# Two pairs of casts on ScalarE and one normalisation on VectorE, moved to other places in a fused attention and expert kernel

## The reference

```
attn_out = softmax(mask(q k^T / 8)) v          # 4 x 8 heads, 576 positions, head size 64, mask by blocks of 64
x = attn_out as 2304 tokens x 512
p = domain_probs / (domain_probs.sum(-1) + 1e-9)     # 2304 x 4
for e in range(4):
    h = max(x @ w1[e], 0)                      # 2304 x 1024
    out += p[:, e:e+1] * (h @ w2[e])           # 2304 x 512
h = out @ w_in; solu = h * softmax(h); ln = layernorm(solu) * g_ln
return ln @ w_out                              # 2304 x 512
```

## Time and profile before

| what | value |
|---|---|
| median of 3 runs | 1162.6 us (1162.32 to 1163.42) |
| the profiled execution's own time | 1163.42 us |
| its span | 1161.6 us |
| PE busy | 1141.0 us (98%) |
| PEld busy | 1020.3 us (88%) |
| DVE busy | 643.9 us (55%) |
| ACT busy | 425.7 us (37%) |
| POOL busy | 415.1 us (36%) |
| longest wait of PE | 2.9 us, for the sum of line 1412 |

### The profile page before, as it was taken

One profiled execution on the slowest core, in us unless ns is written; L12 is line 12 of the kernel. 1 busy time (PEld: TensorE's weight loads), 2 busy tenths in 40 slices (PEclk: granted clock), 3 DMA queues, 4 the chain that ended last, 5 costly groups with the idle time before them and its releaser, 6 DMA issues.

```text
span 1161.6 us, 16745 instructions
## 1 busy us (share of the span) xinstructions
PE 1141.0 (98%) x6131; PEld 1020.3 (88%) x6131; DVE 643.9 (55%) x1155; ACT 425.7 (37%) x927; POOL 415.1 (36%) x403
## 2 busy tenths in 40 slices
PE   8999998989999999999999999999999999999998
PEld 7999898879999999999999999999999977888887
DVE  8999997544343534343433434352424468666765
ACT  7888785232213311113311112321112344434432
POOL 7998896753335100014300004500002463432330
PEclk9999999999999999999999999999999999999999
DMA  4766676983743322162505052513126100000000
GB/s 141 219 201 200 215 237 198 368 327 137 251 165 121 124 82 109 53 210 59 206 1 190 1 209 84 192 42 113 79 82 199 37 19 10 28 19 28 19 28 37
DMA packets 68341, 146.28 MB, mean 126 GB/s; under 512 B 6064, under 2 KB 34736, under 8 KB 68272
## 3 DMA queue, kind: packets, MB, share of 16 engines
q1 hardware_dynamic: 68272, 145.36, 36.1%
HBM read 114.60 MB, written 30.74 MB: 125 GB/s over the span
## 4 chain that ended last, share of the span: by engine, by line
PE 76%; POOL 1%; DVE 1%; DMA 1%; ACT 0%; issue 0%; SPq 0%; ACTq 0%; POOLq 0%
PE s L1721 34%; PE outp L1582 19%; PE s L1582 11%; PE ring L1582 10%; PE ring L1852 1%; DMA xr<-x_stash 1%; PE s L1795 1%; POOL x_late L761 0%; DMA x_stash<-x_tmp 0%; POOL yop_l L863 0%; DVE yop_l L1430 0%; ACT y_t L1100 0%; DVE acc L1376 0%; POOL x_tmp L785 0%; DVE ex L1502 0%
## 5 line engine op out<-in xcount | busy, mean ns | idle before, releaser
L1721 PE MATMUL s<-xr,w1s 128*128 128x384 f32 x2016 | 361.1, 337 | 4.9 <-DVE u L1412 3.1
L1721 PEld LDWEIGHTS s<-xr,w1s 128*128 128x128 f32 x2016 | 351.9, 189 | 10.0 <-DVE u L1412 3.7
L1053 ACT ACTIVATE hid_h<-u 128x384 fp32r<-128x384 f32 x96 | 50.4, 525 | 372.5 <-DVE u L1407 346.7
L720 POOL TENSOR_TENSOR work<-work 128x256 f32<-128x256 f32 x20 | 15.9, 797 | 393.5 <-DMA work<-in_moe_w 268.8
L1362 DVE SCALAR_TENSOR_TENSOR hid_l<-s,hid_h 128x384 fp32r<-128x384 f32 x48 | 26.7, 557 | 125.5 <-ACT hid_h L1049 125.5
L1721 PE MATMUL s<-w1s,yop_h 128*128 128x512 f32 x252 | 85.8, 399 | 1.8 <-POOL yop_l L863 0.7
L1319 DVE TENSOR_TENSOR u<-s,m_b 128x384 f32<-128x384 f32 x24 | 13.4, 557 | 131.9 <-PE s L1721 131.9
L1049 ACT ACTIVATE hid_h<-s 128x384 fp32r<-128x384 f32 x48 | 23.5, 490 | 154.6 <-PE s L1582 154.6
L1582 PE MATMUL s<-k_h,qb 128*128 128x288 f32 (+8 forms) x320 | 76.0, 325 | 2.4 <-ACT pr L906 1.3
L906 ACT ACTIVATE pr<-s,neg_max 128x576 f32<-128x576 f32 (+2 forms) x144 | 75.5, 533 | 5.1 <-DVE neg_max L1198 4.8
L1582 PE MATMUL outp<-w_h,hid_h 128*128 128x512 f32 x192 | 75.5, 393 | 0.0
(11 more groups left out here) (172 smaller groups left out, 2455.6 us busy)
## 6 DMA issues: line engine op xcount, KB each, us to landing
xr<-x_stash SPq DMA_DIRECT2D x77, 768.0 KB, 6.4
r_sb<-r_scratch SPq DMA_DIRECT2D x16, 576.0 KB, 4.3
x_rows<-x_n SPq DMA_DIRECT2D x32, 288.0 KB, 4.6
work<-x_rows SPq DMA_DIRECT2D x24, 384.0 KB, 6.7
x_stash<-x_tmp SPq DMA_DIRECT2D x12, 768.0 KB, 3.8
work<-in_moe_w SPq DMA_DIRECT2D x32, 256.0 KB, 4.2
stage<-in_moe_w SPq DMA_DIRECT2D x32, 256.0 KB, 5.2
x_stash<-xr SPq DMA_DIRECT2D x7, 768.0 KB, 10.7
```

What stands on the lines that cost most here:

```text
L720: pool.tensor_tensor(s1, a21, a22, ALU.add).then_inc(w1_sums, 1)
L1053: act.activation(hid[slot][0][:, :], source, ACT.Relu).then_inc(hid_high, 1)
L1721: last = pe.matmul(target, x, y, start=start and i == 0, stop=stop and i == 2, skip_group_check=True)
```

## The change

In unit 2 (e = 0, sg = 0, u = 2) and unit 6 (e = 0, sg = 1, u = 2), the casts of rounds 0 and 1 of half 1 of the next group are taken from their place behind c11 and put behind c12, the last activation of the unit. The same casts of half 0, in units 1 and 5, stay where they are. `normalise_probs` goes from unit 2 to unit 1.

```diff
@@ after_c11(e, sg, u), ScalarE
-                if e == 0 and sg < 2 and u in (1, 2):
-                    x_cast(sg + 1, u - 1, 0)
-                    x_cast(sg + 1, u - 1, 1)
+                if e == 0 and sg < 2 and u == 1:
+                    x_cast(sg + 1, 0, 0)
+                    x_cast(sg + 1, 0, 1)
@@ unit(e, sg, u), ScalarE
                 hid_rest(m, "c12", 3, u2[:, :])
+                if e == 0 and sg < 2 and u == 2:
+                    x_cast(sg + 1, 1, 0)
+                    x_cast(sg + 1, 1, 1)
@@ unit(e, sg, u), VectorE
-                if m == 2:
+                if m == 1:
                     normalise_probs()
```

## The result

| | before | after |
|---|---|---|
| median | 1162.67 us (1162.32 to 1163.42) | 1172.3 us (1171.28 to 1173.45) |
| profiled execution | 1163.42 us | 1173.69 us |
| span | 1161.6 us | 1171.9 us |
| PE busy | 1141.0 us | 1143.4 us |

The ratio is 1.0083, 95% interval [1.0064, 1.01]: slower by 9.6 us. The forecast was +6.3 us, 1168.9 (1166.1 to 1171.6). The sign was right; the time lies 0.7 us outside the range.

What follows compares the result with a forecast made beforehand. TensorE, busy 1141.0 of 1161.6 us, was taken as the bound, with unit 4's m2 load taking up unit 2's gain. Terms 0 + 0.1 + 5.5 + 0.7 = +6.3 us gave 1168.9 us, range 1166.1 to 1171.6.

Steps and rivals of the forecast that it cites:

- `normalise_probs`: Unit 1: the moved normalisation fits VectorE's gap before u3 and costs nothing; value 0, bounds 0 and +1 us.
- The clock at unit 4: Unit 4: the wait before m1 may lower the clock, but slow products end near 257.0; value 0, bounds 0 and +1.5.
- Unit 2: +0.1: Units 2 to 4: the c12 wait goes, but its 4.4 us goes into waiting for unit 4's m2 load; +0.1 us.
- Unit 6: +5.5: Units 6 to 8: later casts delay stores and loads, so m2 of unit 8 starts 5.5 us later; bounds 3.7 and 6.6.
- The copies' waits: Units 3 and 7: TensorE waits 1.1 and 1.2 us for copy_m1 behind the moved casts; unit 7's is within the 5.5.
- Clock at unit 8: Unit 8: load waits bring half clock; m6 hides in the next wait, m2 partly not; +0.7 us, bounds 0 and 1.5.
- Both load waits lower the clock: Rival, units 4 and 8: clock loss of 3.0 us in the sum, total +8.6 us, 1171.2; chance 0.11.
- Shorter chain: Rival, unit 8: store and loads at their fast ends, no clock loss; +3.7 to +4.5 us, about 1166.8; chance 0.22.
- hidden: Rival: unit 8's loads are hidden, leaving only the copy's 1.2 us; 1163.8 us; chance 0.04.
- faster: Rival: unit 2's 4.4 us is kept, less the copies' 1.1 and 1.2; -2.1 us, 1160.5; chance 0.03.

Runs made afterwards that it cites:

- one multiply: The changed kernel with normalise_probs' four multiplies of 18 elements written as one of 72: 1170.77 us, ratio 1.0054 to the kernel before.
- normalisation alone: The kernel before with only normalise_probs moved from unit 2 to unit 1, all casts staying: 1163.52 us, ratio 1.0003.
- unit 2's casts alone: The kernel before with only unit 2's pair of casts moved behind c12: 1164.01 us, ratio 1.0010.
- stores reordered: The kernel before with group 0's operand stores and group 2's first load put later, and GpSimd's join behind two low parts: 1160.19 us, ratio 0.9974.
- that with the normalisation in unit 1: The kernel before with stores reordered, the four multiplies as one, and normalise_probs in unit 1: 1160.28 us, ratio 0.9972.
- unit 6's pair behind the copy: The kernel before with only unit 6's pair of casts moved, behind copy_m1 of unit 7: 1169.85 us, ratio 1.0052.
- unit 6 alone: The kernel before with only unit 6's pair of casts moved behind c12: 1169.60 us, ratio 1.0054.
- stores reordered with one multiply: The kernel before with stores reordered and the four multiplies as one, normalise_probs staying in unit 2: 1160.16 us, ratio 0.9976.
- both pairs: The changed kernel with normalise_probs put back in unit 2, so only both pairs of casts move: 1171.58 us, ratio 1.0075 to the kernel before.
- changed again: The changed kernel run and profiled a second time without any edit: 1172.65 us, ratio 1.0072 to the kernel before.

## Why the prediction was wrong

The chains that the prediction drew were right, but it left one wait out and made one store too short: `normalise_probs` was put at 0 and costs about 1.5 us, and the way to m2 of unit 8 was put at 5.5 and took 6.65. The clock at unit 4, put at 0, is a third and smaller miss. The numbers are those of the two profiles of the changed kernel against before.

**`normalise_probs`: value 0, bounds 0 and +1. This step failed.** It cost 1.5 us of TensorE: the wait of 1.21, and 0.3 for stopping and starting (from m7 of unit 1 to the next row, at 232.41, are 16.98 us, where a quiet unit takes 15.48). The prediction carried durations from one place to another and noted only that "GpSimd is at work beside it in both places". It did ask what twice the time would do, which is nearly what happened, but took off 1 us of room, gave this no value and left it out of its range. The room was not there: u3 starts 2.85 us after m7 of unit 1 instead of 1.24, which is 1.6 us late, and 1.5 of it are lost. The price depends on which GpSimd instruction is beside. In unit 2 before these are adds of 1.0 to 1.3 us, and the multiplies took 0.63, 0.18, 0.88 and 0.18 us; here they are low parts of 1.8 and joins of 1.3. Two single instructions of GpSimd, and of VectorE, in the profile after:

```profile
213.71 1.85 POOL L785 TENSOR_TENSOR x_tmp<-x_late,x_tmp 128x768 fp32r<-128x768 f32 x1
...
216.94 1.27 POOL L761 TENSOR_TENSOR x_late<-work 128x512 f32<-128x512 f32 x1
```
```profile
214.12 1.47 DVE L1360 TENSOR_TENSOR probs_n<-probs_raw,probs_sum 128x18 f32<-128x18 f32 x1
...
217.05 1.20 DVE L1360 TENSOR_TENSOR probs_n<-probs_raw,probs_sum 128x18 f32<-128x18 f32 x1
```

The multiply ends at 215.59, GpSimd's instruction at 215.56; the other pair ends at 218.25 and 218.21. A multiply that takes 0.18 us where nothing is in its way ends when the GpSimd instruction does. The Trainium skill (SBUF — State Buffer, section "Who interferes with whom") says that a VectorE instruction with two SBUF inputs and a GpSimd instruction that reads SBUF exclude each other. These rows agree, and the one multiply, which waits once and not up to four times, is the test. The addition of line 1357 has one input and took longer too: it ended at 213.78, and the low part beside it at 213.75; the sentence on two inputs does not speak of it. The prediction had cited that rule for GpSimd's side alone. That the ends coincide is shown; that the port is the cause is the page's account, and no run here separates it from another one.

And the delay was passed on. With the normalisation alone it was taken up by the wait for c12. With the casts behind c12, they start when TensorE lets them, at 237.79, and so do all the transfers behind: nothing takes it up. In this stage the normalisation alone costs 0.2 us, unit 2's casts alone -0.1, and both together 1.6 to 2.0 us. The first of these is within the scatter named at the table; the last is read against 51.98 and 52.02, which agree.

**Unit 2: +0.1. Right.** The wait for c12 and its slow clock went, the copy's wait is 0.97 (1.1), the low parts take 3.62 us where the earlier trace rows have 3.90, and the casts of unit 2 alone change the stage by -0.1 us in the profile (the medians have +1.2, ratio 1.0010 [1.0000, 1.0020]). All of the 4.4 us that were won at the one place are waited for at the next.

**Unit 6: +5.5, bounds 3.7 and 6.6. Mis-sized: m2 of unit 8 starts 6.65 us later** (at 328.90; 59.35 us after m7 of unit 4, where before it was 318.88 - 266.18 = 52.70). The chain is the forecast one: casts behind c12, low part, first store, third cast, second store, loads. The term that was off is the first store, taken at 3.6 us "at best". The landings of line 555 from 308 us on:

```profile
L555 SPq DMA_DIRECT2D x_stash<-x_tmp x4: 359/360/360, 308.6 to 318.1; - x4
...
DMA to landing us min/median/max: 3.6/4.7/5.6
```

The first took 5.6 us (+2.0), the second in the chain 3.6 instead of the 4.7 assumed (-1.1), and the load for m2 7.9 instead of 7.5 (+0.4). That makes 5.5 + 1.3 = 6.8. The upper bound of 6.6 took 4.7 for that store, the slowest in the earlier trace rows; its 5.6 lay outside that, and the term came out just above its bound. What the long landings have in common stands in the transfers of 308 to 317 us:

```profile
DMA  0000001999999999999999999810000000000000
GB/s 0 0 0 0 0 0 48 355 382 355 389 355 369 362 273 369 376 382 441 362 341 348 355 328 375 301 34 27 20 27 27 20 27 14 0 0 0 0 0 0
...
q8 instruction: 1, 0.02, 0.7%
```

The two stores move at some 360 GB/s until 314 us, and then almost 2 us follow at 20 to 34 GB/s, about a sixteenth of it. That is the rate of one of the 16 DMA engines, so one seems to be behind the others. Beside them falls one packet of the instruction queue, which is 16 KB. The time of this packet, less the time at which the store next to it is issued, goes roughly with the landing in the twelve profiles. That store is the first of the half where unit 6's pair is moved, and the third where it is not.

| packet, us after the issue of the store | that store landed after |
|---|---|
| -1.6 to -0.2 (four: normalisation alone, unit 2 alone, stores reordered, and that with the normalisation in unit 1) | 3.6 us |
| -0.2 to +0.4 (four: unit 6's pair behind the copy, unit 6 alone, stores reordered with one multiply, before) | 4.3 to 4.7 us |
| +3.5 to +3.6 (four: both pairs, one multiply, changed, changed again) | 5.5 and 5.6 us |

The border is not sharp: at -0.18 us (normalisation alone) the store took 3.6, at -0.23 (stores reordered with one multiply) 4.4. Of the four stores of the earlier trace rows two had such a packet beside them and landed after 4.7, so the spread of 3.6 to 4.7 was itself a hint. This is a coincidence in twelve profiles, not an experiment: no kernel moved the packet on purpose, and the last four are also the four that have both pairs moved. What delayed the last part of the store is thus not shown. That it came late is, and it accounts for 0.9 us of the difference between unit 6's pair alone (5.8 us lost) and both pairs (7.6); of the rest the clock is a part.

**The copies' waits: 1.1 and 1.2. Right** (0.97 each), and right that they are part of the 5.5: without it nothing was won.

**Clock at unit 8: +0.7, bounds 0 and 1.5. Within.** Windows of the profile after, and of the changed kernel again (stretch, busy PE PEld DVE ACT POOL, PEclk, DMA share, GB/s):

```profile
257.85:261.37 3.52, 3.52 (x12) 3.42 (x13) 0.56 (x1) 0.00 (x0) 0.00 (x0) 0.58 1.02 426
325.30:328.90 3.60, 3.60 (x12) 3.23 (x12) 0.00 (x0) 0.49 (x1) 0.00 (x0) 0.55 1.01 420
```
```profile
323.75:329.80 6.05, 6.05 (x19) 5.91 (x20) 0.56 (x1) 0.49 (x1) 0.00 (x0) 0.51 1.02 421
```

In the profile after (its second line) m1 and m6 of unit 8 ran at 1.2 GHz inside the wait for m2's load and m2 did not: 6.89 - 6.65 = 0.24 us. In that of the changed kernel again m2 did too, and the stage is 0.9 us longer. **At unit 4: value 0, bounds 0 and 1.5.** There it was 0 to 0.5 us: the changed kernel takes 2.1 and 1.7 us more than unit 2's casts alone from unit 1 to unit 4, of which 1.67 and 1.69 are there when m1 starts. With both pairs alone the clock stayed at 1.00 at unit 4 after 2.38 us of waiting, with one multiply it fell to 0.57 after 2.71, and m7 of unit 4 came 0.9 us later for it.

**The rivals.** "Both load waits lower the clock" had the nearest time (1171.2), and that is luck in part: the clock did fall, at both waits in the first profile, but for some 0.5 us in all, and some 1.1 in the second, not 3.0, and it had no cost for the normalisation either. "Shorter chain" was wrong on the store, "hidden" and "faster" fell with the first profile. The sum by what was measured: 1.5 (u3) + 0.2 (loads of unit 4) + 0.3 (clock there) + 6.65 + 0.24 = 8.9 us in the first profile, 9.4 in the second (1.62 + 7.76), and 9.6 by the medians; the rest is not placed. No case and no end of the range had a cost for the normalisation, and the first store was longer than its upper bound. With the normalisation left in unit 2 the kernel took 1171.58 us, at the very end of the range (1171.6).

## What to carry to other kernels

A duration read at one place of a timeline holds for another only if the neighbours on the other engines are the same instructions: before moving small VectorE instructions, look at how long each GpSimd instruction at the new place is, and count up to one of these for each, or make them one instruction. When work is moved behind something that follows TensorE, every small delay upstream that used to end in a wait for a transfer becomes a cost, so edits that are free alone need not be free together. And where a chain of waits hangs on a store, move the transfers that nobody needs from in front of it, not the work that waits for it: this was worth -3 us where the change cost 9.6.

## What the runs showed of the hardware

- A VectorE multiply of 128x18 took 0.18 us with nothing in its way and 0.63 to 1.77 us beside a GpSimd instruction (1.17 to 1.47 in the changed kernel); one of 128x72 took 1.53 us at the same place. An addition of 128x18 in place took 0.73 us beside a GpSimd instruction of 1.3 us and 1.70 beside one of 1.8.
- A store of 768 KB with nothing ahead of it landed after 3.6 us in four of twelve profiles and after 4.3 to 5.6 us in eight, where a 16 KB packet of the instruction queue started between 0.2 us before its issue and 3.6 us behind it (one of the four had it at 0.2 us before, too). In the changed kernel its last part moved at 20 to 34 GB/s.
- A wait of TensorE costs more than it lasts: one of 1.21 us made the unit 1.5 us longer at full clock, in three profiles (16.96 to 16.98 us from m7 to m7 instead of 15.48).
- Waits of TensorE of 2.57 us (changed kernel) and 2.71 us (one multiply) went with half clock (granted 0.58 and 0.57 in the next matmuls); one of 2.38 us (both pairs, at unit 4) did not (1.00).
